# Gates applied where the first mixture leaves PSUM, and gathers that add to x by themselves

## What is computed

```python
xc = x[do_compute]
e_idx = np.argmax(logits, axis=1)
gate_w = probs[np.arange(len(xc)), e_idx]
for e in range(E):            # E = 8, F = 1024
    mask = e_idx == e
    h = np.maximum(xc[mask] @ w1[e], 0.0)
    y[mask] = gate_w[mask, None] * (h @ w2[e])
out[do_compute] = xc + y
```

```python
for e in range(E):            # E = 4, F = 1024
    h = np.maximum(x @ w1[e], 0.0)
    out += p[:, e:e + 1] * (h @ w2[e])
```

## Time and profile before

| | us |
|---|---|
| runs, three | 777.43, 790.16, 790.33 |
| their median | 790.16 |
| profiled execution, its own time | 778.11 |
| its span, first to last instruction | 776.4 |
| TensorE busy in the span | 743.0 |
| mean granted TensorE clock | 0.986 |

### The profile page before, as it was taken

The page is one execution under the profiler, slowest core; times in us unless marked ns, Lnnn a source line. Parts: engine busy times, 40 slices in busy tenths (PEclk is TensorE's granted clock), DMA queues, the critical chain, the costliest instruction groups (busy, mean ns, idle before and its releaser), DMA issues.

```text
span 776.4 us, 11260 instructions
## 1 busy us (share of the span) xinstructions
PE 743.0 (96%) x4199; PEld 661.5 (85%) x4199; DVE 471.6 (61%) x924; ACT 329.1 (42%) x586; POOL 42.2 (5%) x86
## 2 busy tenths in 40 slices
PE   3999999699999879999999999999999999999998
PEld 2889889488888778998989989989889899898896
DVE  5766666699888587654573475275365265456442
ACT  2666566388988352521432333234144043143230
POOL 3100100110100410000000000000000000000000
PEclk9999999699999999999999999999999999999999
DMA  9569970599990530030021011002003003000112
GB/s 152 101 152 247 291 217 21 199 394 390 390 389 35 156 130 1 1 109 1 0 71 39 1 55 54 1 17 92 0 0 108 0 0 109 0 0 0 41 41 81
DMA packets 86944, 79.28 MB, mean 102 GB/s; under 512 B 50802, under 2 KB 56948, under 8 KB 86900
## 3 DMA queue, kind: packets, MB, share of 16 engines
q1 hardware_dynamic: 81540, 71.32, 29.6%
q0 software_dynamic: 1600, 5.24, 2.2%
q10 hardware_dynamic: 3760, 2.14, 0.9%
HBM read 70.30 MB, written 8.39 MB: 101 GB/s over the span
## 4 chain that ended last, share of the span: by engine, by line
PE 89%; DVE 6%; DMA 2%; issue 1%; ACT 1%; POOL 0%; DVEq 0%; SPq 0%; POOLq 0%
PE ps L1881 32%; PE ps L1858 30%; PE ps L1761 11%; PE ps L1585 3%; PE ps L1610 2%; PE ps L1609 2%; PE ps L1594 2%; PE ps L1565 2%; PE ps L1626 1%; PE ps L1618 1%; PE ps L1736 1%; DVE xs L1448 1%; DVE X L1105 1%; PE ps L1817 1%; DVE ql L1065 1%
## 5 line engine op out<-in xcount | busy, mean ns | idle before, releaser
L1858 PE MATMUL ps<-xs,w1s 128*128 128x384 f32 x1344 | 237.7, 336 | 0.0
L1881 PE MATMUL ps<-w2s,h_hi 128*128 128x512 f32 x768 | 237.1, 390 | 0.6 <-DVE X L1486 0.6
L1858 PEld LDWEIGHTS ps<-xs,w1s 128*128 128x128 f32 x1344 | 235.1, 189 | 1.3
L1881 PEld LDWEIGHTS ps<-w2s,h_hi 128*128 128x128 f32 x768 | 143.7, 188 | 30.2 <-DVE X L1486 1.0
L1881 PE MATMUL ps<-w2s,h_lo 128*128 128x512 f32 x384 | 149.7, 390 | 0.0
L1488 DVE SCALAR_TENSOR_TENSOR X<-ps,prn,X 128x512 f32<-128x512 f32 x84 | 63.1, 751 | 121.7 <-PE ps L1881 121.3
L953 ACT ACTIVATE shared<-ps 128x384 f32<-128x384 f32 x96 | 46.1, 488 | 157.5 <-PE ps L1858 157.3
L1457 DVE TENSOR_TENSOR shared<-ps,shared 128x384 f32<-128x384 f32 x96 | 53.4, 557 | 93.6 <-PE ps L1858 93.3
L1881 PEld LDWEIGHTS ps<-w2s,h_lo 128*128 128x128 f32 x384 | 72.1, 188 | 15.0
L956 ACT ACTIVATE h_hi<-shared 128x384 fp32r<-128x384 f32 x96 | 50.5, 527 | 67.7 <-DVE shared L1457 67.7
L1023 DVE TENSOR_TENSOR piece_lo<-ring,piece_hi 128x1024 fp32r<-128x1024 f32 x48 | 56.4, 1220 | 5.4 <-ACT piece_hi L775 5.4
(11 more groups left out here) (183 smaller groups left out, 798.3 us busy)
## 6 DMA issues: line engine op xcount, KB each, us to landing
ring<-in_moe_w SPq DMA_DIRECT2D x24, 1024.0 KB, 12.3
raw<-in_moe_w SPq DMA_DIRECT2D x16, 1024.0 KB, 5.1
shared<-in_moe_w SPq DMA_DIRECT2D x8, 1024.0 KB, 10.7
X<-in_k SPq DMA_DIRECT2D x16, 192.0 KB, 4.3
shared<-in_q SPq DMA_DIRECT2D x16, 192.0 KB, 4.3
X<-in_v SPq DMA_DIRECT2D x16, 192.0 KB, 3.1
x_d<-X SPq DMA_DIRECT2D x8, 384.0 KB, 3.2
X<-x_d SPq DMA_DIRECT2D x2, 1536.0 KB, 16.5
```

The lines of the kernel that those rows point to most:

```text
L1858: mm = pe.matmul(out_, w1s[:, wp, WI[name], c, f * P:(f + 1) * P], xs[:, 3 * b:3 * b + 3, xp, XI[name], c, :], start=(not onto and x == 0 ...
L1881: mm = pe.matmul(ps[:, 6 + k % 2, :], h_, w2s[:, wp, c, :], start=(x == 0 and c == 0), stop=(x == 2 and c == 3))
```

## The change

1. Gates. gate is stored to g_d in HBM, 1536 single elements, from SyncE's queue behind load_raw1(0) and load_raw2(0). GpSimd waits for it behind the third gather_x and gathers eight columns gate_s, one per expert. y_out waits for four of these (gs_ld) and scales by the gate while it copies. ys_d then holds gated results; the overflow path, which this input doesn't take, does the same.
2. Gathers. The twelve gathers of the seam write no buffer: they add to X (compute_op=ALU.add), each with its own semaphore, and wait for nothing between them. L1812, L1817, diagonal and x2_sum are gone; all tiles are transposed from X.
3. TensorE runs 30 matmuls on constants at the seam ahead of the first tile; w2_high and w2_low of the first unit move behind the first of them.
4. The sums of x2 for the first three pairs are split by kind: S3 first (kind 0), then S1 and S2 (kind 1), then S4 (kind 2), and each product waits for its kind alone.
5. The order of products becomes P1, P2, P7, P4, P6, P5, P3 in all steps, PAIR_BANK changes, and all of the last three pairs' transposes now stand in the outputs of the first step.

```diff
+            sp.wait_ge(route_done, 1)
+                sp.dma_start(g_d.rearrange("(t p) a -> p (t a)", p=P), gate[:, :]).then_inc(gd_st, 16)
@@ gpsimd, behind the first three gather_x
+            pool.wait_ge(gd_st, 16)
+            for e in range(E):
+                pool.indirect_dma_start(gate_s[:, e:e + 1], None, g_d, bass.IndirectOffsetOnAxis(tok_i[:, e:e + 1], 0)).then_inc(gs_ld[e // 4], 16)
@@ gather_y
+                pool.wait_ge(x_ld, 16 * B)
                 for k in range(NT):
-                    if 4 <= k < NFIRST + 4:
-                        pool.wait_ge(x2_tr, k - 3)
-                    elif k >= NFIRST + 4:
-                        pool.wait_ge(x2_sum_done, k - NFIRST - 3)
-                    pool.indirect_dma_start(yg[:, k % 4, :], None, ys_d[0:rows, :],
-                                            bass.IndirectOffsetOnAxis(slot_i[:, TILES[k]:TILES[k] + 1], 0)).then_inc(yg_ld[k % 4], 16)
+                    pool.indirect_dma_start(X[:, TILES[k], :], None, ys_d[0:rows, :],
+                                            bass.IndirectOffsetOnAxis(slot_i[:, TILES[k]:TILES[k] + 1], 0),
+                                            compute_op=ALU.add).then_inc(x2_ld[k], 16)
@@ y_out, scalar
-                act.activation(ysb[e % 2], ps[:, 5 + e % 2, :], ACT.Copy).then_inc(y_cp, 1)
+                act.wait_ge(gs_ld[e // 4], 64)
+                act.activation(ysb[e % 2], ps[:, 5 + e % 2, :], ACT.Copy, scale=gate_s[:, e:e + 1]).then_inc(y_cp, 1)
@@ orders
-        PAIR_BANK = ((4, 1), (5, 2), (6, 7), (6, 7), (1, 2), (4, 5))
+        PAIR_BANK = ((4, 1), (5, 2), (6, 7), (1, 4), (2, 5), (1, 4))
+        KIND = ((5, 6), (3, 5), (6, 7))
+        KIND_OF = {"P7": 0, "P6": 1, "P5": 1, "P3": 2}
-        ITEMS = [(p, f) for p in ("P1", "P2", "P7", "P6", "P4", "P5", "P3") for f in range(2)]
+        ITEMS = [(p, f) for p in ("P1", "P2", "P7", "P4", "P6", "P5", "P3") for f in range(2)]
@@ tensor, the seam
-            pe.wait_ge(x_ld, 32)
+            for x in range(30):
+                mm = pe.matmul(ps[:, 0, :].rearrange("p (a c) -> p a c", c=P), ones_b[:, :],
+                               ident_b[:, :].unsqueeze(1).broadcast_to([P, 4, P]), start=True, stop=True)
+            def tile_transposed(k):
+                pe.wait_ge(x2_ld[k], 16)
+                for c in range(KD):
+                    mm = pe.transpose(ps[:, tile_bank(k), c * P:(c + 1) * P], X[:, TILES[k], c * P:(c + 1) * P], ident[:, :])
+                mm.then_inc(x2_tr, 1)
@@ tensor, outputs
-                    if begin and k < 2:
-                        pe.wait_ge(added, 6)
-                        x2_transposed(4 + k)
+                    if begin and k < 3:
+                        x2_transposed(3 + k)
@@ scalar, ahead of the first step
+            act.wait_ge(x2_begun, 1)
+            for j in range(2):
+                w2_high(0, 0, j)
             x2_high(0)
             x2_high(1)
-            s_high(0)
+            kind_high(0, 0)
+            kind_high(1, 0)
             x2_high(2)
-            s_high(1)
-            s_high(2)
+            kind_high(2, 0)
+            kind_high(0, 1)
+            kind_high(1, 1)
+            kind_high(0, 2)
+            kind_high(1, 2)
@@ vector, ahead of the first step
             s_sums(1)
-            s_low(0)
-            s_sums(2)
-            s_low(1)
-            s_low(2)
-            x2_sum(6)
-            x2_sum(7)
+            s_sum(2, 0)
+            for p in range(3):
+                kind_low(0, p)
+            s_sum(2, 1)
+            s_sum(2, 2)
+            s_sum(2, 3)
+            for p in range(3):
+                kind_low(1, p)
```

More of the change, by code:

```diff
@@ L396, in build @@
         ov_st = sem("ov_st")
-        yg_ld = [sem(f"yg_ld{j}") for j in range(4)]
-        dg_done = sem("dg_done")
-        x2_sum_done = sem("x2_sum_done")
+        gd_st = sem("gd_st")
+        gs_ld = [sem(f"gs_ld{j}") for j in range(2)]
+        x2_ld = [sem(f"x2_ld{k}") for k in range(NT)]
         x2_tr = sem("x2_tr")
@@ L404, in build @@
         s_made = sem("s_made")
+        x2_begun = sem("x2_begun")
         s_hi = sem("s_hi")
         s_lo = sem("s_lo")
+        kind_hi = [sem(f"kind_hi{g}") for g in range(3)]
+        kind_lo = [sem(f"kind_lo{g}") for g in range(3)]
         raw1_ld = sem("raw1_ld")
@@ L921, in _ @@
                         piece_high(b + 3, x)
[L922 to L927, removed]
+                if b == 29:
                     w1_high(0, 0, 0)
@@ L948, in s_high, with kind_high, step @@
                                xs_f[:, p, 1, 3:7, :].rearrange("p a c -> p (a c)"), ACT.Copy).then_inc(s_hi, 1)
-            def step(m, half, b, inserted=None):
+            def kind_high(g, p):
+                i, j = KIND[g]
+                if g < 2:
+                    act.wait_ge(s_step, 3 * p + (1, 3)[g])
+                else:
+                    act.wait_ge(s_made, p + 1)
+                act.activation(xs[:, p, 0, i:j, :, :].rearrange("p a k c -> p (a k c)"),
+                               xs_f[:, p, 1, i:j, :].rearrange("p a c -> p (a c)"), ACT.Copy).then_inc(kind_hi[g], 1)
+            def step(m, half, b, begin=False):
                 def copy(item, slot, f):
@@ L959, in step @@
                     copy(0, 0, f)
+                if begin:
+                    for f in range(2):
+                        copy(4, 1, f)
                 wait(act, m2y, by_step(m, half, b, 6, 0))
@@ L963, in step @@
                     hidden(part[:, 0, f, :], f, 0)
[L964 to L967, removed]
+                if begin:
+                    kind_high(2, 1)
+                    kind_high(2, 2)
+                else:
+                    for f in range(2):
+                        copy(4, 1, f)
                 for f in range(2):
                     act.wait_ge(hd_lo, by_step(m, half, b, 8, 1 + f))
-                    copy(6, 0, f)
+                    copy(8, 0, f)
                 for f in range(2):
@@ L983, in m2_units @@
                     begin = first and not half
-                    for j in range(2):
-                        w2_high(m, half, j)
                     if begin:
-                        step(m, half, 0, lambda: x2_high(3))
+                        step(m, half, 0, True)
+                        x2_high(3)
+                        x2_high(4)
                         s_high(3)
-                        x2_high(4)
                         x2_high(5)
@@ new lines, in s_sums, with kind_low @@
+            def s_sums(p):
+                for i in range(4):
+                    s_sum(p, i)
+            def kind_low(g, p):
+                i, j = KIND[g]
+                dve.wait_ge(kind_hi[g], p + 1)
+                if g:
+                    dve.wait_ge(s_made, p + 1)
+                here = xs_f[:, p, 1, i:j, :].rearrange("p a c -> p (a c)")
+                dve.tensor_tensor(xs[:, p, 1, i:j, :, :].rearrange("p a k c -> p (a k c)"), here,
+                                  xs[:, p, 0, i:j, :, :].rearrange("p a k c -> p (a k c)").bitcast(F32), ALU.subtract).then_inc(kind_lo[g], 1)
@@ L1493, in m2_units, with middle @@
                     if begin:
[L1494 to L1498 removed]
+                        def middle():
+                            for p in range(3):
+                                kind_low(2, p)
                         step(m, half, 0, middle)
[L1501 to L1503 removed]
                         outputs(m, half, 0, 0, True)
+                        x2_low(3)
+                        outputs(m, half, 0, 1, True)
+                        s_sums(3)
+                        outputs(m, half, 0, 2, True)
                         x2_low(4)
                         s_sums(4)
[L1507 removed]
+                        outputs(m, half, 0, 3, True)
                         x2_low(5)
                         s_sums(5)
+                        outputs(m, half, 0, 4, True)
+                        s_low(3)
                         s_low(4)
[L1511 removed]
+                        outputs(m, half, 0, 5, True)
                         s_low(5)
[L1513 to L1514 removed]
                     else:
@@ L1534, in _ @@
             dve.wait_ge(x_ld, 32)
+            for j in range(2):
+                w2_low(0, 0, j)
             x2_low(0)
@@ L1860, in products @@
                     mm.then_inc(prod, 1)
-                    if begin and b == 0 and (name, f) == ("P2", 1):
-                        x2_transposed(3)
             def outputs(m, half, b, first):
```

99 lines of the change are left out of this document (45 added, 54 removed).

## The result

| | before | after |
|---|---|---|
| runs, us | 777.43, 778.10, 790.16, 790.33 | 792.59, 793.13, 793.67, 793.88 |
| median, us | 784.13 | 793.4 |
| profiled execution, us | 778.11 | 793.67 |
| its span, us | 776.4 | 791.6 |
| mean granted TensorE clock | 0.986 | 0.974 |

The changed kernel is slower: 1.0189 times the time before by the record, with an interval of 1.0177 to 1.0201; against the two lower times of this table it is 1.020. Two of the four times before are some 12 us above the other two, and the ratio leaves them out. The forecast of 786 us had the chain of causes and not the size.

The account below looks back on a forecast made before the run. TensorE was taken as the bound, busy 743.0 of 776.4 us. From 778.1, late gates add 10.9 us, the seam gives back 3.1 and the new order costs zero: 785.9, say 786 us; range 773 to 800.

Parts of the forecast that it names:

- Step a: SyncE's queue: the gates' store of 1536 elements, behind both weight loads, takes 4.1 us and lands at 171.0 us.
- Step b: GpSimd: eight gathers of gates behind the store, 1.5 us apart, 4.5 us to land; first four there at 180.1.
- Step c: ScalarE's y_out(0) waits for gates and delays the relu; TensorE stalls 9.2 us, plus 1.7 us for low clock.
- Step d: GpSimd's gather_x(3) queues behind the gates' gathers, 6.0 us hidden by the other stall; piece loads have 11 us cover.
- Part 2: At the seam, adding gathers 2.0 us apart and removed work gain 3.1 us; ends: 5.5 gain, 4.0 loss.
- Part 3: P4 right behind P7 in all sixteen steps: margin 0.45 us to P7's copy, so cost zero.
- the latest rival: First mixture: store written at 178.7 us, gates there at 190.7, TensorE stalls 19.8 us, total 796; chance 0.12.
- The gates come in time: First mixture: store overtakes queued loads or gathers land at once; no stall, 773 to 775 us; chance 0.18.
- The adding gathers are slow: Seam: tiles 3.2 us apart from reading twice, seam loses 4.0 us, total 793; chance 0.15.
- The gates come much later: First mixture: store written at 178.7 us, gathers land in 7.4, stall 19.8 us, total 796; chance 0.12.
- P4 misses: Second mixture: P4 misses its copy by 0.2 us in each of 16 steps, total 789; chance 0.05.
- The 0.50: Whole kernel: the chance given to the forecast case itself, a time of 781 to 791 us.

## Why the prediction was wrong in size

**Step a, the store: the term that failed.** The order was right: the elements' packets begin behind the first load's landing (164.4), and the store lands behind both loads. The price wasn't. It landed at 175.33 us and not at 171.0; counted from the predicted 166.9 that is 8.4 us for 1536 elements where 4.1 was taken, and inside the stated ends of 2.9 and 11.8. The row it was sized by was a load of 1536 pieces that landed after 5.9 us, a load and not a store, issued at 1.9 us of the span; the engines weren't idle there either (share 0.47 over 2 to 5 us, 1.38 over 5 to 8), so traffic beside it may not be the difference, and whether writing is wasn't tested. It also delayed the load ahead of it: raw2 landed at 172.9, not 166.9. Placed first it took 15.7 us, on another queue 19.5. The price followed the store's form, not its 6 KB. The packets themselves began within 3 us, near the 4.1 that was taken; the 8 us behind the last of them stood in no row.

**Step b, the gathers of gates.** Issued 1.25 us apart, not 1.5; landing 5.82 us, not 4.5. Together 0.6 us more than predicted, with 0.16 more before the first. In other runs issues of 1.3 to 4.84 us appear, so the 3.07 us of before's gather was no outlier; here, with the other engines standing, none was over 0.95.

**Step c, who waits.** Right, to 0.1 us: with the gates there at 185.2, the formula gives 185.2 - 169.47 - 1.68 = 14.1 us (169.47 is before's start plus the 0.25 by which this execution was later), and the hole is 14.06. The low clock cost between 1.38 us, read directly, and the 1.68 that the sum leaves; predicted 1.7.

**Step d, what else is queued.** Right that gather_x(3) is hidden by the other stall, and that it would cost by itself; the 6.0 us it was given grow with the store to 12.33. That the first wait is little worth removing alone (a stall of 9.2 us against 6.0 behind it) stood in the prediction's numbers, but was not drawn from them; at the measured size it was worth nothing. No wait for a piece load shows on TensorE: the cover of 11 us held.

**Part 2, the seam.** Gain 1.14 us, predicted 3.1. The spacing was right: gathers start 1.85 us apart and tiles come 2.1 us apart on TensorE (277.20 to 287.65, five steps), predicted 2.0, with ends at 1.6 and 3.2. The first tile was the miss: 5.92 us from the start of its gather (271.28 to 277.20), where 3.9 was taken from the 3.5 of before. Its issue alone took 2.35 us instead of 0.95. (A plain first gather took 1.80 us with the gates left out, so not all of that is the adding.) The products began 17.1 us after the first gather, not 14.8; from there to the second step it took 35.1, predicted 35.4. The stall of 1.25 us at P4 didn't come: the chain has the 84 products without a break. They last 15.63 instead of 14.60, with the clock at 0.50 until 290.9; that low stretch was in no term, and the slower products may have hidden the stall. TensorE's timeline has the tiles and the clock, 1.1 us for four transposes:

```profile
277.20 1.11 PE L1859 MATMUL ps<-ident,X 128*128 128x128 f32 x4 [3.42 <-DMA X<-ys_d,slot_i]
279.83 1.11 PE L1859 MATMUL ps<-ident,X 128*128 128x128 f32 x4 [1.52 <-DMA X<-ys_d,slot_i]
281.82 1.09 PE L1859 MATMUL ps<-ident,X 128*128 128x128 f32 x4 [0.87 <-DMA X<-ys_d,slot_i]
```

The outputs with three pairs of transposes last 19.1 us (304.37 to 323.51), predicted 19.45.

**Part 3.** Predicted zero, measured +0.35 over fifteen steps, and +0.19 with the order alone.

**The sum.** From 785.9 to the 793.67 of the profiled execution: +4.9 for the stall (store +4.3, its gathers +0.6), +2.0 for the seam, +0.35 for the steps, +0.25 for the later start, and 0.36 more around the span. The prediction's own sums hold to 0.5 us (the latest rival adds up to 796.5, not 796). The time lay inside the range of 773 to 800, near that rival and not near the forecast. Against the profiled 778.11 the forecast was 1.0% slower and 2.0% came; against the median of 790.16 that stood beside it, 786 was a gain, and no gain came.

**The rivals.** "The gates come in time" fell, in its overtaking form too. "The adding gathers are slow" fell: tiles 2.1 us apart, not 3.2. The cost behind it is there all the same. The Trainium skill puts a reduce at about half a copy's rate ("Collectives: The Full Stack", Why ReduceScatter is half of AllGather). Per share of the engines these gathers agree, 145 against 302 GB/s; the time didn't double because plain gathers had left a third of the engines free. "The gates come much later" was the nearest: it gave 796, with gates at 190.7 where they came at 185.2. "P4 misses" fell. The 0.50 lay on a case whose store sat 1.2 us above its lower end and 7.7 below its upper one; the row nearest to it in load, the full engines of rows 4, should have pulled it to the upper half.

## What to carry to other kernels

Look at how many pieces a small store has, not at its bytes: transpose on chip until the last dimension is contiguous. 6 KB in 1536 elements beside full DMA engines took 15.7 to 20.8 us from issue to landing, in 12 rows about 7.4. When something comes late, list every queue that waits behind it: two stalls hid each other here, one wait taken away gave nothing, and the time came back only with its cause, the store. A gather that adds takes 0.6 us more of GpSimd's issue time and about twice the engines' time per byte; use it where tiles aren't waited for one by one.

## What the runs showed of the hardware

Matmuls at a lower rate without a lower granted clock. The profiled execution of the kernel with the gates left out took 789.37 us, its other executions mostly 778 to 780. Windows of 30 to 40 us, first the kernel before (profiled at 778.11), then the kernel with the gates left out:

```profile
30.00:40.00 10.00, 9.79 (x91) 8.84 (x90) 7.55 (x28) 6.29 (x16) 1.66 (x4) 1.00 0.29 65
```

```profile
30.00:40.00 10.00, 10.00 (x52) 9.42 (x51) 4.44 (x17) 4.24 (x10) 0.00 (x0) 1.00 0.00 0
```

TensorE does 52 matmuls where it did 91, although the granted clock of the rows is 1.00 in both. From 25 to 51 us a pair of matmuls of attention (L1646 there, L1610 before) takes 0.63 us instead of 0.39; what follows runs as before, 11 us late. The profile without fillers (789.27) has the same row, x52 at 1.00. The changes don't touch this stretch. What causes it stays open. The 790.16 and 790.33 us of before, for which the prediction widened its range, have the fitting size, but were not profiled.

A store of elements holds up more than itself, and longest after its packets have begun: 1568 packets under 512 B in 3 us, then 14 GB/s (167 to 172 us) at a DMA share of 0.44, with 2 KB packets of the loads taking up to 5.5 us. On another queue it interleaves with the loads nearly packet by packet (1630 small among 3451) instead. Neither tells which part of a transfer the engines wait for.

Adding gathers: 2368 packets where plain ones have 1600, for the same 5.24 MB, and 3.4% of the engines' time over the span where plain ones take 2.3%.
